# Splitting the queries on GpSimd ahead of the transposes, in an attention and MLP chain on one Trainium2 core

## What is computed

```python
# attention, for each of 32 heads
scores = (q @ k.T) / 8
cum = cumsum(maximum(s, 0))
scores = where(causal, -1e9, scores + minimum(-(cum[:, None] - cum[None, :]), 0))
attn = softmax(scores)
x = attn @ v                       # heads side by side: [4, 576, 512]
# first MLP
xn = (x - mean) / sqrt(var + 1e-6) * g_ln
x = x + maximum(xn @ w_ch1, 0) @ w_ch2
# second step: mix over positions by U (576x32), V (32x576), then an MLP
u = x + (x.T @ U @ V).T
out = u + maximum(u @ w_ch1b, 0) @ w_ch2b
```

## Time and profile before

| what | value |
|---|---|
| median of 3 runs | 1116.96 us (1113.01 to 1121.07) |
| the profiled execution's own time | 1115.07 us |
| its span in the profile | 1113.3 us |
| its mean granted TensorE clock | 0.992 |
| busy over the span: PE, DVE, ACT, POOL | 1051.2, 811.7, 557.2, 339.6 us |

### The profile page before, as it was taken

How to read it: one execution, slowest core, us unless ns; L and a number is a source line. 1 busy time by engine, 2 the same in 40 slices (tenths; PEclk the granted TensorE clock), 3 DMA queues, 4 the chain that set the end, 5 groups by cost and what they waited for, 6 DMA issues and landing times.

```text
span 1113.3 us, 21040 instructions
## 1 busy us (share of the span) xinstructions
PE 1051.2 (94%) x6936; PEld 931.8 (84%) x6936; DVE 811.7 (73%) x1732; ACT 557.2 (50%) x1265; POOL 339.6 (31%) x377
## 2 busy tenths in 40 slices
PE   6788888888797999999999999999999999999998
PEld 5677777777687898889888889888889888888887
DVE  6899999999558768767767757976865866765532
ACT  5788888888444344444444434443423432433321
POOL 1154453211116433333324232333232423332100
PEclk9999999999898999999999999999999999999999
DMA  5745545445241321322231343432142133223131
GB/s 155 233 120 132 126 120 130 127 119 159 83 134 64 108 76 57 123 68 77 76 114 58 114 151 107 156 112 82 62 138 96 66 100 121 75 84 114 58 127 44
DMA packets 156260, 118.71 MB, mean 107 GB/s; under 512 B 86496, under 2 KB 131552, under 8 KB 156192
## 3 DMA queue, kind: packets, MB, share of 16 engines
q1 hardware_dynamic: 156192, 117.80, 35.2%
HBM read 98.82 MB, written 18.95 MB: 106 GB/s over the span
## 4 chain that ended last, share of the span: by engine, by line
PE 89%; DVE 3%; ACT 3%; issue 2%; DMA 1%; SPq 1%; POOL 0%; ACTq 0%; DVEq 0%; POOLq 0%
PE ps_up L751 9%; PE ps_up L752 9%; PE ps_up L753 9%; PE ps_acc L798 6%; PE ps_acc L797 6%; PE ps_acc L799 6%; PE ps_s L798 5%; PE ps_s L797 5%; PE ps_s L799 5%; PE ps_x L681 5%; PE ps_s L651 3%; PE ps_pt L662 3%; ACT prob L928 2%; PE ps_up L662 2%; PE ps_up L627 2%
## 5 line engine op out<-in xcount | busy, mean ns | idle before, releaser
L751 PE MATMUL ps_up<-z,w 128*128 128x256 f32 x896 | 255.6, 285 | 4.7 <-DVE z L1270 3.8
L752 PE MATMUL ps_up<-z,w 128*128 128x256 f32 x896 | 254.4, 284 | 0.0
L753 PE MATMUL ps_up<-z,w 128*128 128x256 f32 x896 | 254.4, 284 | 0.0
L564 POOL TENSOR_TENSOR w_f<-raw 128x256 f32<-128x256 f32 x64 | 69.0, 1078 | 412.1 <-DMA raw<-in_moe_w_ch 397.4
L751 PEld LDWEIGHTS ps_up<-z,w 128*128 128x128 f32 x896 | 172.3, 192 | 10.6 <-DVE z L1270 4.2
L752 PEld LDWEIGHTS ps_up<-z,w 128*128 128x128 f32 x896 | 172.5, 193 | 5.1
L753 PEld LDWEIGHTS ps_up<-z,w 128*128 128x128 f32 x896 | 172.8, 193 | 0.0
L797 PE MATMUL ps_acc<-w_hi,h 128*128 128x512 f32 x320 | 126.7, 396 | 1.9 <-DVE x_res L1296 1.9
L798 PE MATMUL ps_acc<-w_lo,h 128*128 128x512 f32 x320 | 126.8, 396 | 0.0
L799 PE MATMUL ps_acc<-w_hi,h 128*128 128x512 f32 x320 | 126.2, 394 | 0.0
L1093 ACT ACTIVATE h<-cs 128x768 fp32r<-128x768 f32 x64 | 54.1, 846 | 126.8 <-DVE cs L1383 126.8
(11 more groups left out here) (170 smaller groups left out, 2642.7 us busy)
## 6 DMA issues: line engine op xcount, KB each, us to landing
raw<-in_moe_w_ch SPq DMA_DIRECT2D x80, 512.0 KB, 3.6
ncum_b<-ncum_dram SPq DMA_DIRECT2D x32, 288.0 KB, 3.5
x_in<-x_dram SPq DMA_DIRECT2D x18, 512.0 KB, 4.3
k_raw<-in_k SPq DMA_DIRECT2D x64, 128.0 KB, 2.5
u_dram<-x_in SPq DMA_DIRECT2D x9, 512.0 KB, 2.8
q_raw<-in_q SPq DMA_DIRECT2D x32, 128.0 KB, 3.2
v_raw<-in_v SPq DMA_DIRECT2D x32, 128.0 KB, 2.2
w_f<-in_moe_w_ch SPq DMA_DIRECT2D x4, 1024.0 KB, 8.1
```

What stands on the lines that cost most here:

```text
L564: pool.tensor_tensor(to[:, I5, 1], a21, a22, ALU.add).then_inc(s1_done, 1)
L751: nc.tensor.matmul(bank, w_hi, z_hi, start=(start and c == 0), stop=False, skip_group_check=True)
L752: nc.tensor.matmul(bank, w_hi, z_lo, start=False, stop=False, skip_group_check=True)
L753: last = nc.tensor.matmul(bank, w_lo, z_hi, start=False, stop=(stop and c == 1), skip_group_check=True)
```

## The change

GpSimd gets a new function, `split_queries(u)`. It waits for the load of the queries and for `qt_done` of the head before, then writes the high half (a multiply by one) and the low half (a subtract) side by side into a new tile `q_split` of 128 partitions x 4 tiles x 2 halves x 64. It is called for heads 0 and 1 ahead of everything else of the attention, and for head u + 2 at the head of turn u, ahead of `split_values(u)`. TensorE transposes `q_split`, both halves at once, 128 columns, into 128 partitions; ScalarE copies all 128 partitions in one instruction. VectorE's `q_low` is gone. `load_q` now waits on `q_lo_done`, GpSimd's low half, since that is what reads `q_raw` last. Keys and last tiles are as before.

```diff
+            q_split = sbuf("q_split", [P, QT - 1, 2, D], F32R, small)
...
             def load_q(u):
 
-                wait(sp, qt_done, u)
+                wait(sp, q_lo_done, u)
                 sp.dma_start(q_raw[:], flat_rows(q_f, u)).then_inc(q_loaded, 16)
...
+            def split_queries(u):
+
+                pool.wait_ge(q_loaded, 16 * u + 16)
+                waits_apart(pool, (qt_done, u))
+                pool.tensor_tensor(q_split[:, :, 0, :], q_raw[:], one[:].unsqueeze(2).to_broadcast([P, QT - 1, D]), ALU.mult).then_inc(q_hi_done, 1)
+                pool.wait_ge(q_hi_done, u + 1)
+                pool.tensor_tensor(q_split[:, :, 1, :], q_raw[:], q_split[:, :, 0, :].bitcast(F32), ALU.subtract).then_inc(q_lo_done, 1)
...
+            split_queries(0)
+            split_queries(1)
             pool.wait_ge(pads_done, 1)
             for u in range(HEADS):
+                if u + 2 < HEADS:
+                    split_queries(u + 2)
                 split_values(u)
...
-                waits_apart(pe, (q_loaded, 16 * u + 16), (l_lo_done, u))
-
-                bank = up[0][0:D, :].rearrange("d (n t) -> d t n", t=QT - 1)
+                waits_apart(pe, (q_lo_done, u + 1), (l_lo_done, u))
+
+                bank = up[0].rearrange("d (n t) -> d t n", t=QT - 1)
                 for t in range(QT - 1):
-                    last = nc.tensor.transpose(bank[:, t], q_raw[:, t], ident)
+                    last = nc.tensor.transpose(bank[:, t], twice(q_split[:, t]).bitcast(F32), ident)
...
-                    pe.wait_ge(q_lo_done, u + 1)
+                    pe.wait_ge(q_done, u + 1)
...
             def q_high(m, p):
                 act.wait_ge(qt_done, 2 * m + p + 1)
-                nc.scalar.activation(q2s[p][0:D, 0:FULL], up[0][0:D, 0:FULL], ACT.Copy, scale=-SCALE).then_inc(q_hi_done, 1)
+                nc.scalar.activation(q2s[p][:, 0:FULL], up[0][:, 0:FULL], ACT.Copy, scale=-SCALE).then_inc(q_done, 1)
...
-            def q_low(m, p):
-                dve.wait_ge(q_hi_done, 2 * m + p + 1)
-                q2 = q2s[p]
-                nc.vector.scalar_tensor_tensor(out=q2[D:P, 0:FULL], in0=up[0][0:D, 0:FULL], scalar=-SCALE,
-                                               in1=q2[0:D, 0:FULL].bitcast(F32), op0=ALU.mult, op1=ALU.subtract).then_inc(q_lo_done, 1)
```

More of the change, by code:

```diff
@@ L231, in chain_kernel @@
         qt_done, kt_done, lt_done = sem("qt_done"), sem("kt_done"), sem("lt_done")
-        q_hi_done, q_lo_done = sem("q_hi_done"), sem("q_lo_done")
+        q_hi_done, q_lo_done, q_done = sem("q_hi_done"), sem("q_lo_done"), sem("q_done")
         k_hi_done, k_lo_done = sem("k_hi_done"), sem("k_lo_done")
@@ L1201, in head_alone @@
                     weights_low(0)
-                if more:
-                    q_low(*second(m, p))
                 if not final:
@@ L1342, in prepare @@
                     second_low(j)
-            q_low(0, 0)
             k_low(0, 0)
@@ L1348, in _ @@
                 bias_and_max(0, 0, i)
-            q_low(0, 1)
             k_low(0, 1)
```

## The result

The changed kernel takes 1131.74 us (median of 4 runs, 1131.07 to 1133.84), the kernel before 1116.84. The ratio is 1.013, with a 95% interval of 1.0098 to 1.0162: slower by some 15 us, or 1.3%. The profiled execution took 1131.99 us with a span of 1130.2, 16.9 more than the span before.

A forecast was written before the change was run, and what follows sets the result against it. The prediction took the TensorE, ScalarE, TensorE chain as the bound, VectorE beside it; the change closes a slower ring. 26 x 0.47 = 12.2 plus 1.4 at the start, 13.6 on 1115.07, gives 1129 us, range 1115 to 1139.

The forecast's parts named there:

- The ring sets the pace: Attention loop: value split, SyncE's issues, query landing and query split close a turn of 8.82 us, +0.47 us a head.
- Its terms: Ring's parts: value split 1.66, signal 0.24, issues 2.06, landing 3.2, landing to GpSimd's start 0.24, query split 1.42 us.
- The landing: Query load from issue to arrival: 3.2 us, the median of 24, with the sums' 288 KB issued just ahead.
- VectorE's freed time is worth 0: Removing the 684 ns q_low from VectorE in each head gains 0, at most 0.48 us a head.
- The guess from the slices: Attention stage, slices 3 to 10: VectorE, nine tenths busy, is the bound and whatever leaves it pays in full.
- the chain: Attention heads: the path that ended last runs TensorE, ScalarE, TensorE, without VectorE's instruction of the queries.
- The wider transposes at +0.15 us a head: TensorE's query transposes, 128 columns for 64, take 0.59 for 0.44 us; a head takes 8.5 if nothing else binds.
- a rival at 1120: Attention loop: the ring has slack and only the wider transposes are felt, 28 x 0.15 = 4.2 us; chance 0.27.
- TensorE waits 0.3 us a head for the split: At each head's query transposes TensorE waits some 0.3 us for GpSimd's q_split, 8.82 less 8.5.
- The start at 1.4 us, going through nearly whole: Attention's start: first queries pass GpSimd 1.66 us before TensorE; taken as 1.4 us of the total, bounds 0 and 1.7.
- the 13.6 of the forecast: Whole kernel: 12.2 us from 26 turns of the ring plus 1.4 at the start, added to 1115.07 us.
- had weighed it for the loop: Rival: GpSimd slowed beside VectorE, its split pair 2.0 for 1.42 us, a further 15 us, 1144; chance 0.08.

The follow-up runs named there:

- run 1: Changed kernel with SyncE issuing the query load ahead of the value load: 1117.11 us against 1118.05 for the kernel before, ratio 1.0009.
- run 2: Changed kernel with the query load ahead of the sums' load only, still behind the values: 1117.73 us, ratio 0.9995 to the kernel before.
- run 5: Changed kernel, its order of loads kept, with the multiply of GpSimd's query split done twice: 1160.28 us, ratio 1.0407 to the kernel before.
- run 6: Kernel of run 1 with the same doubled GpSimd multiply as run 5: 1117.48 us, ratio 1.0011 to the kernel before.
- run 4: Kernel before without VectorE's low halves of the queries, left out of the first 512 queries' scores: 1117.88 us, ratio 0.9998.
- Run 3: Kernel before with only the query transposes widened from 64 to 128 columns: 1118.64 us, ratio 1.0004.
- run 7: Kernel of run 1 with the query copy moved from ScalarE to VectorE: 1116.82 us, ratio 1.0 to the kernel before.
- run 10: Kernel before with TensorE transposing probabilities 3 first, ScalarE's query copy behind exponential 4, VectorE's q_low behind probabilities 3's low half: 1119.28 us, ratio 1.0006.

## Why the prediction was right, point by point

*The ring sets the pace: right.* The prediction named a ring of 8.82 us a head and a pair of 17.6; the trace has 8.70 as the mean of the 23 turns at full clock (8.40 to 9.17) and a pair of 17.57 in the turn shown. Runs 1 and 2 open or shorten it and the loss goes; run 5 lengthens it by 0.69 and the turns at full clock grow by 0.68; run 6 shows that the same work outside it is free.

*Its terms.* The split of the queries was put at 0.617, 0.726 and a gap, 1.42 in all: 618 and 733 ns. The landing stayed at 3.2, and the cause given (the sums' 288 KB ahead) is shown by run 2. From query issue to GpSimd's start it is 3.63 in the turn shown, where 3.2 + 0.24 were taken. The whole is 0.12 short of the estimate as a mean over 23 turns. That little counts, since only what the ring exceeds the heads by is paid: 0.34 a turn in place of 0.47, 8.8 us in place of 12.2.

*VectorE's freed time is worth 0: right*, and shown by run 4 alone. The guess from the slices (nine tenths busy, so the bound) was wrong and the chain was right.

*The wider transposes at +0.15 us a head: wrong.* Run 3 says 0. The step took a time on the chain from another place in the order as if it were the price of the form. It didn't reach the sum, since the ring was the longer, but it made a rival at 1120, which with 0 and the ring open is 1117 (run 1).

*TensorE waits 0.3 us a head for the split: right as a mean.* The weight load ahead of these transposes waits 7.3 us in some 22 heads, 0.33 a head, but unevenly: the matmul waits 0.15 to 0.81 us in 13 of the heads and not at all in the others, among them the three right behind a fall of the clock.

*The start at 1.4 us, going through nearly whole: wrong.* VectorE's first row maximum starts at 13.14, where the earlier trace rows have 10.81, 2.3 later. The 1.66 that were added ahead of the first transposes were 2.5, through the multiply of 1.52 beside VectorE's scan. But with the ring open the same delay (13.06 in run 1) is made good by head 3. In the changed kernel 3.3 us are lost up to there, with the ring closed and with a fall of the clock that run 1 doesn't have; the prediction counted nothing for the ring in these heads.

*A term was missing:* the falls of TensorE's clock, 3.7 us in the loop and an unknown part of the 3.3 ahead of it. Without the 3.7 the trace has 8.8 + 3.3 + 1.1 = 13.2 us, beside the 13.6 of the forecast, but that closeness is luck: the ring's part was forecast 3.4 too high, and what came ahead of the loop's turns and behind them was 4.4 in place of 1.4. What is earned is the ring itself, its length to 0.12 us and that it sets the pace.

## What to carry to other kernels

An engine with idle time isn't free if its work stands between a load and the release of the next one: follow the order of issue on the DMA queue round until it comes back to where it began, and add up one turn. When a turn of such a ring comes out near the period of the loop, try moving one load ahead of the wait of another: here it cost nothing and took the ring out. And where removing work from the fullest engine brings nothing, look for a second path of equal length: here leaving out VectorE's low half (run 4), taking the copy off ScalarE (run 7) and the new orders (run 10) were each worth 0, and together they were worth 18 to 19 us.

## What the runs showed of the hardware

**TensorE's clock.** With TensorE waiting once more in about every second head (0.15 to 0.81 us), the granted clock fell from 1.00 to 0.50 for some 3 us in three heads of the loop, and these heads took 1.24 us more. Each of the three falls came within a microsecond of the end of TensorE's wait of 1.08 us for the exponential. With longer waits (run 5) the mean over 200 us was 0.91. In run 1, with the same work and without the added waits, it was 1.00. So here the falls go with the added waits, which cost more than their own length. Which wait brings a fall isn't shown: the longest of the changed kernel, 0.81 us at 244.64, was followed by none, and the kernel before, with a wait of 1.1 us in each head, had none in the loop.

**GpSimd beside VectorE.** A multiply of 128x256 took 1.52 us, 1.1 of them beside a scan of two SBUF operands, and 0.61 without:

```profile
3.34 1.35 DVE L1128 TENSOR_TENSOR_SCAN ncum<-ones,s_rows 32x576 f32<-32x576 f32 x1
...
3.58 1.52 POOL L549 TENSOR_TENSOR q_split<-q_raw,one 128x256 fp32r<-128x256 f32 x1 [1.63 <-DMA q_raw<-in_q]
```

This is the changed kernel's timeline. Beside VectorE's instructions in the loop, of which the large ones have one operand in PSUM, the same multiply held 618 ns as a mean over 25 heads. It is the contention that the Trainium skill states (GPSIMD Engine Reference, Specifications: the SBUF interface is shared, and VectorE instructions with two SBUF inputs contend). That section gives no size; here GpSimd lost 0.9 us in 1.1 us of overlap. The prediction had weighed it for the loop, where it didn't show, and missed it at the start, where it did.
